# Two VectorE passes of a rational feed-forward stage joined over pairs of groups, with six buffers in place of four

## The chip, the cores and the metric

The kernel runs on one core of one Trainium2 chip. The metric is the time of one execution on the device, in microseconds (us). Of the core's engines TensorE (PE in the profile) multiplies matrices, VectorE (DVE) and ScalarE (ACT) work element by element, GpSimd (POOL) does so as well and also issues some of the DMAs, and SyncE (SP) issues the others.

## The reference, cut to what matters

The input has 4 x 3008 tokens of 256 values. A Fourier transform along the tokens, a complex 256x256 mix with a soft threshold, and the inverse transform come first. Each of the 12032 resulting tokens then goes through a feed-forward layer whose activation is a quotient of two polynomials:

```python
h = x @ w_in                       # 256 -> 2048
P = a[0] + a[1]*h + a[2]*h**2 + a[3]*h**3
Q = 1.0 + abs(b[0])*abs(h) + abs(b[1])*h**2
g = P / (Q + 1e-06)
out = g @ w_out                    # 2048 -> 256
```

## The kernel before

The feed-forward layer is cut into 26 tiles of 470 tokens (the last has 282). Each tile has eight groups, and a group is 256 of the 2048 hidden values, held as 128 partitions x 940 numbers. Groups are numbered through, 0 to 207. Every engine runs a loop over slots `q`; a slot handles one group at each step, and different steps of one slot belong to different groups. Each engine's order is written out by hand, and semaphores tie the engines together.

The steps of group r are these:

- PE, `group_f1` (L541): 12 matmuls at L552 make h in PSUM, in one of two buffers. It runs in PE's slot r-2 and waits for `n_n3` of group r-2, since VectorE must be done with that buffer.
- ACT, `group` (L770), in ACT's slot r-1: `den` = |h| scaled (L776), `sq` = h squared, scaled (L779), `num` (L782). The first waits until the remainder of group r-4 is done (`n_rest`), the second until `g_lo` of group r-4 is done (`n_g`), as the buffers come round after four groups.
- POOL, `tail` (L1135): a DMA adds `sq` to `den` (L1140). In ACT's slot r, L846 and L849 turn the sum into 1/Q, which goes into `sq`.
- DVE, in its slot r: L1087 and L1090 finish the numerator but for its constant. Both read h from PSUM. In slot r+1, `rounded` (L1056, its operation at L1062) makes `g_hi`, the quotient rounded to the format of the second matmul.
- DVE, in slot r+2: `multiplied` (L1065, at L1067) makes g_hi times the denominator, in `den`. `remainder` (L1071, at L1073) subtracts that from the numerator, in `num`. The order in a slot q is L1087 and L1090 for q, L1067 for q-2, L1062 for q-1, L1073 for q-2.
- POOL, in slot r+3: `g_lo` = num x sq (L1148), after the DMA of group r+3 in POOL's order and before that of group r+4.
- PE, in slot r+3: `group_f2_hi` (L567, L569) and `group_f2_lo` (L582) add g_hi and g_lo times w_out. `g_hi` has three buffers and `g_lo` two.

Up to about slot 141 the engines also carry the rest of the transform. PE has L469 to L493 for that. ACT has L722, L739 (`below`, which makes `neg`) and L750. DVE has `lower_x` (L945, L948), `soft` (L954, which reads `neg` and stands after L1073 in even slots), and twice a chain of small operations on the scales (slots 88 and 142). In the slots 1 and 3 of each tile PE does the last inverse step at L529. ACT reads it a slot later, at L762, or at L759 in the last tiles. `split_lo` (L1022) follows on DVE.

## Time and profile before

| | |
|---|---|
| median of 3 runs | 1445.55 us (1444.42 to 1447.71) |
| profiled execution | 1446.29 us, of which its span is 1444.1 us |
| busy share of the span | PE 96%, DVE 92%, ACT 87%, POOL 44% |
| mean granted TensorE clock | 0.991 |

The busy shares are over the whole span, and the stages have different limits. The prediction therefore reads two stretches by themselves. The first is DVE's slots 80 to 142, from 674.87 to 1081.37 us, in which the transform's work still runs. The second is slots 143 to 197, from 1081.37 to 1389.00 us, with the feed-forward layer and the inverse step alone. A slot starts where L1087 starts. In the timeline the columns are the start in us, the duration in us, the engine, line and operation, what it writes and reads with its size, and in brackets the idle time before it with what ended it. A waiting matmul or operation is shown from its start on, so a wait inside an operation makes it longer.

### The profile page before, as it was taken

How to read it: one execution, taken by the hardware profiler on the slowest of the kernel's cores; microseconds unless marked ns; L12 is line 12 of the kernel's file. 1: busy time of each engine (PE TensorE's matmuls, PEld its weight loads, DVE VectorE, ACT ScalarE, POOL GpSimd, SP SyncE). 2: the span in 40 equal slices, each digit the busy share in tenths (PEclk: the TensorE clock that was granted, in tenths of full speed). 3: DMA queues.
4: the chain of work that ended last, by engine and by line, in shares of the span. 5: the costliest groups of instructions: out<-in, count | busy, mean ns of one | idle time of the engine just before them, and what ended most of it. 6: DMA issues, size and time to landing. Idle time of an engine off the chain costs nothing.

```text
span 1444.1 us, 21576 instructions
## 1 busy us (share of the span) xinstructions
PE 1391.0 (96%) x7498; PEld 974.2 (67%) x7498; DVE 1333.8 (92%) x1650; ACT 1251.6 (87%) x1657; POOL 632.8 (44%) x417
## 2 busy tenths in 40 slices
PE   7998999999999999999999999999999999999987
PEld 2776667677666676776767776776766666666666
DVE  5576989989999999999999999999999999999998
ACT  3577989988989889888889989988989999999986
POOL 0000544444445444444445445545445555555554
PEclk8999999999999999999999999999999999999999
DMA  8885666666456656555555555555545555555443
GB/s 260 250 266 142 146 156 138 135 140 150 102 118 154 146 112 140 128 115 122 121 108 127 121 113 118 129 111 111 114 109 108 107 94 112 117 108 110 86 97 70
DMA packets 97913, 188.07 MB, mean 130 GB/s; under 512 B 11216, under 2 KB 57744, under 8 KB 97808
## 3 DMA queue, kind: packets, MB, share of 16 engines
q0 software_dynamic: 29952, 98.58, 36.8%
q1 hardware_dynamic: 67856, 88.12, 20.7%
q8 instruction: 62, 1.02, 0.3%
q14 instruction: 43, 0.35, 0.1%
HBM read 50.60 MB, written 37.49 MB: 61 GB/s over the span
## 4 chain that ended last, share of the span: by engine, by line
PE 53%; DVE 19%; ACT 16%; issue 8%; DMA 2%; POOL 1%; SPq 0%; ACTq 0%; DVEq 0%; POOLq 0%
PE h_ps L552 18%; PE o_ps L582 6%; PE o_ps L567 6%; PE o_ps L569 6%; DVE den L1067 4%; DVE num L1073 4%; DVE num L1087 4%; DVE g_hi L1062 4%; PE d L529 3%; ACT num L782 3%; ACT sq L779 3%; ACT den L776 3%; ACT sq L846 3%; PE d L493 2%; PE o_ps L463 2%
## 5 line engine op out<-in xcount | busy, mean ns | idle before, releaser
L1148 POOL TENSOR_TENSOR g_lo<-num,sq 128x940 fp32r<-128x940 f32 (+1 forms) x205 | 469.5, 2290 | 99.7 <-DVE num L1073 99.5
L1140 POOL DMA_DIRECT2D den<-sq x208 | 182.8, 879 | 698.9 <-ACT sq L779 369.0
L567 PE MATMUL o_ps<-g_hi,wout_hi 128*128 128x470 f32 (+1 forms) x832 | 342.1, 412 | 0.9 <-DVE g_hi L1062 0.9
L569 PE MATMUL o_ps<-g_hi,wout_lo 128*128 128x470 f32 (+1 forms) x832 | 310.5, 374 | 0.0
L552 PE MATMUL h_ps<-yt_hi,win_hi 128*128 128x470 f16 (+1 forms) x832 | 301.9, 363 | 5.3 <-DVE num L1090 5.3
L552 PE MATMUL h_ps<-yt_hi,win_lo 128*128 128x470 f16 (+1 forms) x832 | 300.1, 361 | 0.0
L552 PE MATMUL h_ps<-yt_lo,win_hi 128*128 128x470 f16 (+1 forms) x832 | 300.1, 361 | 0.0
L1087 DVE TENSOR_TENSOR num<-h_ps,num 128x940 f32<-128x940 f32 (+1 forms) x208 | 232.1, 1116 | 33.8 <-ACT num L782 33.0
L1090 DVE SCALAR_TENSOR_TENSOR num<-num,coef,h_ps 128x940 f32<-128x940 f32 (+1 forms) x208 | 245.2, 1179 | 7.4
L1067 DVE SCALAR_TENSOR_TENSOR den<-den,g_hi 128x940 f32<-128x940 f32 (+1 forms) x208 | 244.2, 1174 | 0.1
L1062 DVE SCALAR_TENSOR_TENSOR g_hi<-num,a_sb,sq 128x940 fp32r<-128x940 f32 (+1 forms) x208 | 244.3, 1174 | 0.0
L1073 DVE SCALAR_TENSOR_TENSOR num<-num,a_sb,den 128x940 f32<-128x940 f32 (+1 forms) x208 | 244.2, 1174 | 0.1
L779 ACT ACTIVATE sq<-h_ps,coef 128x940 f32<-128x940 f32 (+1 forms) x208 | 214.8, 1033 | 27.4 <-POOL g_lo L1148 26.2
L582 PE MATMUL o_ps<-g_lo,wout_hi 128*128 128x470 f32 (+1 forms) x832 | 213.8, 379 | 21.8 <-POOL g_lo L1148 21.0
L782 ACT ACTIVATE num<-h_ps,coef 128x940 f32<-128x940 f32 (+1 forms) x208 | 234.5, 1127 | 0.0
L846 ACT ACTIVATE sq<-den,qone 128x940 f32<-128x940 f32 (+1 forms) x208 | 223.8, 1076 | 3.9 <-DMA den<-sq 3.8
L776 ACT ACTIVATE den<-h_ps,coef 128x940 f32<-128x940 f32 (+1 forms) x208 | 213.2, 1025 | 5.8 <-DVE num L1073 4.2
L849 ACT ACTIVATE sq<-sq 128x940 f32<-128x940 f32 (+1 forms) x208 | 203.2, 977 | 6.6
L582 PEld LDWEIGHTS o_ps<-g_lo,wout_hi 128*128 128x128 f32 x832 | 152.2, 189 | 56.5 <-POOL g_lo L1148 37.6
L567 PEld LDWEIGHTS o_ps<-g_hi,wout_hi 128*128 128x128 f32 x832 | 157.9, 190 | 30.9 <-issue 8.3
L569 PEld LDWEIGHTS o_ps<-g_hi,wout_lo 128*128 128x128 f32 x832 | 158.0, 190 | 23.5 <-issue 7.5
L552 PEld LDWEIGHTS h_ps<-yt_hi,win_hi 128*128 128x128 f16 x832 | 81.2, 98 | 115.4 <-issue 47.9
(161 smaller groups left out, 1581.1 us busy)
## 6 DMA issues: line engine op xcount, KB each, us to landing
den<-sq POOLq DMA_DIRECT2D x200, 470.0 KB, 4.4
spec<-s1w SPq DMA_DIRECT2D x64, 192.0 KB, 2.8
z_in<-spec SPq DMA_DIRECT2D x96, 128.0 KB, 2.6
spec<-s_out SPq DMA_DIRECT2D x96, 128.0 KB, 1.9
xw<-in_x SPq DMA_DIRECT2D x31, 384.0 KB, 4.8
out_t<-o_sb SPq DMA_DIRECT2D x25, 470.0 KB, 4.2
zp_in<-spec SPq DMA_DIRECT2D x22, 480.0 KB, 5.4
inv_in<-in_inv SPq DMA_DIRECT2D x96, 64.0 KB, 2.3
```

The lines of the kernel that those rows point to most:

```text
L552: mm = pe.matmul(h_ps[q % 2][:, j, 0:cols(q)], w[:, h, f * P:(f + 1) * P], y[t % 2][:, h, 0:cols(q)], start=i == 0, stop=i == len(terms) - 1)
L567: pe.matmul(o_ps[:, h, 0:w], wout_hi[:, f, h * P:(h + 1) * P], g_hi[q % 3][:, j, 0:w], start=f == 0, stop=False)
L569: mm = pe.matmul(o_ps[:, h, 0:w], wout_lo[:, f, h * P:(h + 1) * P], g_hi[q % 3][:, j, 0:w], start=False, stop=False)
L582: mm = pe.matmul(o_ps[:, h, 0:w], wout_hi[:, f, h * P:(h + 1) * P], g_lo[q % 2][:, j, 0:w], start=False, stop=f == FB - 1)
L779: act.activation(ring(sq, q), h, ACT.Square, scale=scales(q // SLOTS, 3)).then_inc(n_sq, 1)
L782: act.activation(ring(num, q), h, ACT.Identity, bias=scales(q // SLOTS, 4), scale=scales(q // SLOTS, 5)).then_inc(n_num, 1)
L846: act.activation(ring(sq, q), ring(den, q), ACT.Abs_reciprocal_sqrt, bias=qone[:, 0:1]).then_inc(n_rs, 1)
L1062: dve.scalar_tensor_tensor(out=g_hi[r % 3][:, :, 0:w], in0=ring(num, r), scalar=a_sb[:, 0:1], in1=ring(sq, r), op0=ALU.add, op1=ALU.mult). ...
L1067: dve.scalar_tensor_tensor(out=ring(den, r), in0=ring(den, r), scalar=1.0 + 1e-6, in1=g_hi[r % 3][:, :, 0:cols(r)].bitcast(F32), op0=ALU.a ...
L1073: dve.scalar_tensor_tensor(out=ring(num, r), in0=ring(num, r), scalar=a_sb[:, 0:1], in1=ring(den, r), op0=ALU.add, op1=ALU.subtract).then_ ...
L1087: dve.tensor_tensor(top, h, top, ALU.mult).then_inc(n_n2, 1)
L1148: pool.tensor_tensor(g_lo[r % 2][:, :, 0:cols(r)], ring(num, r), ring(sq, r), ALU.mult).then_inc(n_g, 1)
```

## The change

For the groups 80 to 197 (`PAIRED`), L1067 and L1073 become one operation each for two groups, an even one and the next odd one, with 1880 numbers in each partition. The product of the pair r, r+1 stands at the end of DVE's slot r+2, behind `rounded(r+1)`, whose result it reads, and behind `split_lo` and `soft`. The remainder of the pair stands in slot r+3, after L1090 and `lower_x` and before `rounded(r+2)`. The second matmul and `g_lo` of a paired group come one slot later, in slot r+4. `num`, `den` and `sq` have six buffers from group 80 on. Two of each lie in the space of the inputs `x` and of the first transform's output, which are no longer used by then; two waits check this. `g_hi` has four buffers in place of three for all groups. A small start-up buffer is shared with `neg`, and `pick` becomes bf16.

```diff
+PAIRED = range(80, 198)
 def f2_slot(r):
+    if r in PAIRED:
+        return r + 4
     return r + 3 if late(r) else r + 2
+def place(q):
+    return q % 4 if q < PAIRED[0] else (q - PAIRED[0] + 4) % 6
...
-                done = [r for r in (q - 3, q - 2) if 0 <= r < NS and f2_slot(r) == q]
+                done = [r for r in (q - 4, q - 3, q - 2) if 0 <= r < NS and f2_slot(r) == q]
...
-                if q >= 4:
-                    act.wait_ge(n_rest, q - 3)
+                before = user_before(q)
...
+                if before is not None:
+                    act.wait_ge(n_rest, back_steps(before))
...
-                if r >= 3:
-                    dve.wait_ge(f2h, r - 2)
+                if r >= 4:
+                    dve.wait_ge(f2h, r - 3)
...
+            def multiplied_pair(r):
+                dve.wait_ge(n_hi, r + 2)
+                dve.scalar_tensor_tensor(out=both(den_pairs, r), in0=both(den_pairs, r), scalar=1.0 + 1e-6,
+                                         in1=g_hi_pairs[r // 2 % 2][:, :, :].bitcast(F32),
+                                         op0=ALU.add, op1=ALU.mult).then_inc(n_back, 1)
+            def remainder_pair(r):
+                dve.wait_ge(n_back, back_steps(r))
+                dve.scalar_tensor_tensor(out=both(num_pairs, r), in0=both(num_pairs, r), scalar=a_sb[:, 0:1],
+                                         in1=both(den_pairs, r), op0=ALU.add, op1=ALU.subtract).then_inc(n_rest, 1)
...
-                if 0 <= q - 2 < NS and late(q - 2):
+                if 0 <= q - 2 < NS and late(q - 2) and q - 2 not in PAIRED:
                     multiplied(q - 2)
...
+                if q - 3 in PAIRED and q % 2 == 1:
+                    remainder_pair(q - 3)
                 if 0 <= q - 1 < NS:
                     rounded(q - 1)
...
+                if q - 2 in PAIRED and q % 2 == 0:
+                    multiplied_pair(q - 2)
...
-                for r in [r for r in (q - 3, q - 2) if 0 <= r < NS and f2_slot(r) == q and not on_vector(r)]:
-                    pool.wait_ge(n_rest, r + 1)
+                for r in [r for r in (q - 4, q - 3, q - 2) if 0 <= r < NS and f2_slot(r) == q and not on_vector(r)]:
+                    pool.wait_ge(n_rest, back_steps(r))
```

## Rows read from the trace of the kernel before

**Rows 1.** Busy time by stretch; columns: stretch, length, engines' busy time, clock, DMA share, GB/s.
```profile
674.87:1081.37 406.50, 399.84 (x2215) 287.03 (x2213) 392.73 (x481) 360.92 (x452) 194.53 (x126) 1.00 0.54 117
1081.37:1389.00 307.63, 297.39 (x1457) 197.04 (x1458) 305.03 (x277) 287.86 (x310) 170.24 (x110) 0.99 0.53 105
```

**Rows 2.** Chain that ended last, shares by line, 674.87 to 1081.37 us.
```profile
by line: PE h_ps L552 24.2%; PE o_ps L582 8.7%; PE o_ps L567 8.5%; PE o_ps L569 8.4%; issue 5.9%; PE d L529 4.8%; ACT num L782 4.0%; ACT den L776 3.9%; ACT sq L779 3.7%; ACT sq L846 3.4%; PE d L469 2.0%; PE d L493 1.9%; DVE num L1073 1.7%; 
```

**Rows 3.** The same, 1081.37 to 1389.00 us.
```profile
by line: issue 15.9%; DVE den L1067 13.4%; DVE num L1073 13.0%; DVE g_hi L1062 12.6%; DVE num L1087 12.2%; PE h_ps L552 6.8%; POOL g_lo L1148 4.3%; ACT num L782 4.0%; ACT sq L779 3.8%; ACT den L776 2.8%; PE o_ps L582 2.7%; PE d L529 2.1%; A
```

**Rows 4.** Timeline of DVE, slot 168 and the start of 169.
```profile
1221.39 1.13 DVE L1087 TENSOR_TENSOR num<-h_ps,num 128x940 f32<-128x940 f32 x1
1222.55 1.19 DVE L1090 SCALAR_TENSOR_TENSOR num<-num,coef,h_ps 128x940 f32<-128x940 f32 x1
1223.66 1.13 DVE L1067 SCALAR_TENSOR_TENSOR den<-den,g_hi 128x940 f32<-128x940 f32 x1
1224.71 1.19 DVE L1062 SCALAR_TENSOR_TENSOR g_hi<-num,a_sb,sq 128x940 fp32r<-128x940 f32 x1
1225.82 1.19 DVE L1073 SCALAR_TENSOR_TENSOR num<-num,a_sb,den 128x940 f32<-128x940 f32 x1
1226.92 1.13 DVE L1087 TENSOR_TENSOR num<-h_ps,num 128x940 f32<-128x940 f32 x1
```

**Rows 5.** Groups of DVE by shape, from 1081.37 us; last column: busy us, mean ns.
```profile
L1073 DVE SCALAR_TENSOR_TENSOR num<-num,a_sb,den 128x940 f32<-128x940 f32 x60 | 71.4, 1190 | 0.0
L1073 DVE SCALAR_TENSOR_TENSOR num<-num,a_sb,den 128x564 f32<-128x564 f32 x8 | 6.4, 797 | 0.1
```

**Rows 6.** Timeline of POOL in slot 168.
```profile
1221.56 2.22 POOL L1148 TENSOR_TENSOR g_lo<-num,sq 128x940 fp32r<-128x940 f32 x1 [0.82 <-DVE num L1073]
1225.41 0.88 POOL L1140 DMA_DIRECT2D den<-sq  x1 [1.63 <-PE o_ps L582]
```

**Rows 7.** Timeline of PE in slot 168: L582, first and last matmul of L552.
```profile
1223.83 1.12 PE L582 MATMUL o_ps<-g_lo,wout_hi 128*128 128x470 f32 x4 [0.30 <-POOL g_lo L1148]
1224.79 0.37 PE L552 MATMUL h_ps<-yt_hi,win_hi 128*128 128x470 f16 x1
...
1226.98 0.36 PE L552 MATMUL h_ps<-yt_hi,win_lo 128*128 128x470 f16 x1
```

**Rows 8.** Timeline of ACT in slot 168.
```profile
1222.24 1.03 ACT L776 ACTIVATE den<-h_ps,coef 128x940 f32<-128x940 f32 x1
1223.81 1.05 ACT L779 ACTIVATE sq<-h_ps,coef 128x940 f32<-128x940 f32 x1 [0.54 <-POOL g_lo L1148]
```

**Rows 9.** Timeline of POOL near 538 us.
```profile
537.92 0.90 POOL L1140 DMA_DIRECT2D den<-sq  x1 [5.25 <-issue]
538.53 2.51 POOL L1148 TENSOR_TENSOR g_lo<-num,sq 128x940 fp32r<-128x940 f32 x1
```

**Rows 10.** Timeline of DVE near 540 us.
```profile
540.00 2.05 DVE L1067 SCALAR_TENSOR_TENSOR den<-den,g_hi 128x940 f32<-128x940 f32 x1
```

**Rows 11.** Timeline of DVE at a tile's slot 4, in the second stretch.
```profile
1201.31 1.33 DVE L1067 SCALAR_TENSOR_TENSOR den<-den,g_hi 128x940 f32<-128x940 f32 x1
```

**Rows 12.** Timeline of ACT at a tile's slot 4, in the first stretch.
```profile
861.00 0.48 ACT L739 ACTIVATE neg<-d,x_lam 128x256 f32<-128x256 f32 x1
```

**Rows 13.** Timeline of DVE in the same slot, 108, and the next.
```profile
861.60 0.42 DVE L954 SCALAR_TENSOR_TENSOR ythr<-d,neg 128x256 f32<-128x256 f32 x1 [0.35 <-ACT neg L739]
...
862.63 1.14 DVE L1087 TENSOR_TENSOR num<-h_ps,num 128x940 f32<-128x940 f32 x1 [0.59 <-ACT num L782]
```

**Rows 14.** Timeline of PE: the first L552 of slot 109.
```profile
866.42 0.37 PE L552 MATMUL h_ps<-yt_hi,win_hi 128*128 128x470 f16 x1
```

**Rows 15.** Waits in the first stretch; columns: us in total, times, longest.
```profile
PEld d L529 <- ACT s_out L750: 6.3, 8, 2.0
```

**Rows 16.** Timeline of PE in slot 83: the first L567 and the first L552.
```profile
694.68 0.46 PE L567 MATMUL o_ps<-g_hi,wout_hi 128*128 128x470 f32 x1
...
697.33 0.37 PE L552 MATMUL h_ps<-yt_hi,win_hi 128*128 128x470 f16 x1
```

More of the change, by code:

```diff
@@ L158, in on_vector, with back_steps, user_before @@
     return r >= NS - 3
+PAIRED = range(80, 198)
 def f2_slot(r):
+    if r in PAIRED:
+        return r + 4
     return r + 3 if late(r) else r + 2
+def back_steps(r):
+    pairs = sum(1 for s in PAIRED if s % 2 == 1 and s < r)
+    return r + 1 - pairs - (r in PAIRED and r % 2 == 1)
+def place(q):
+    return q % 4 if q < PAIRED[0] else (q - PAIRED[0] + 4) % 6
+def user_before(q):
+    if q < PAIRED[0]:
+        return q - 4 if q >= 4 else None
+    return q - 6 if q >= PAIRED[0] + 2 else None
 LATE_TILES = range(ENTRY[-1], NT)
@@ L237, in spectral_ffn @@
         neg = sb("neg", P, D)
+        bias_rest = neg
         ythr, s4_out = several("ythr", 2, P, D), several("s4_out", 2, P, D)
@@ L240, in spectral_ffn @@
         yt_hi, yt_lo = several("yt_hi", 2, P, KH, 480, dt=F16), several("yt_lo", 2, P, KH, 480, dt=F16)
-        num, sq, den = (several(n, 4, P, GB * BANK) for n in ("num", "sq", "den"))
-        g_hi, g_lo = several("g_hi", 3, P, GB, TOK, dt=F32R), several("g_lo", 2, P, GB, TOK, dt=F32R)
+        num_pairs, den_pairs = [several(n, 2, P, 2, GB * BANK) for n in ("num", "den")]
+        num_pairs.append(xw[:, 0:2, :, :].rearrange("p i a d -> p i (a d)"))
+        den_pairs.append(xw[:, 2:4, :, :].rearrange("p i a d -> p i (a d)"))
+        num, den = ([pair[:, i, :] for pair in pairs for i in range(2)] for pairs in (num_pairs, den_pairs))
+        sq = [t[:, :] for t in several("sq", 4, P, GB * BANK)]
+        sq += [s1w[:, 2 * i:2 * i + 2, :].rearrange("p i d -> p (i d)") for i in range(2)]
+        g_hi_pairs, g_lo = several("g_hi", 2, P, 2, GB * TOK, dt=F32R), several("g_lo", 2, P, GB, TOK, dt=F32R)
+        g_hi = [pair[:, i, :].rearrange("p (j n) -> p j n", j=GB) for pair in g_hi_pairs for i in range(2)]
         o_sb = several("o_sb", 2, P, KH, TOK)
@@ L301, in ring, with both @@
         def ring(tiles, q):
-            return tiles[q % 4][:, 0:GB * cols(q)].rearrange("p (j n) -> p j n", j=GB)
+            return tiles[place(q)][:, 0:GB * cols(q)].rearrange("p (j n) -> p j n", j=GB)
+        def both(pairs, q):
+            return pairs[place(q) // 2][:, :, 0:GB * cols(q)]
         zp_count = []
@@ L566, in group_f2_hi @@
                     for h in range(KH):
-                        pe.matmul(o_ps[:, h, 0:w], wout_hi[:, f, h * P:(h + 1) * P], g_hi[q % 3][:, j, 0:w],
+                        pe.matmul(o_ps[:, h, 0:w], wout_hi[:, f, h * P:(h + 1) * P], g_hi[q % 4][:, j, 0:w],
                                   start=f == 0, stop=False)
-                        mm = pe.matmul(o_ps[:, h, 0:w], wout_lo[:, f, h * P:(h + 1) * P], g_hi[q % 3][:, j, 0:w],
+                        mm = pe.matmul(o_ps[:, h, 0:w], wout_lo[:, f, h * P:(h + 1) * P], g_hi[q % 4][:, j, 0:w],
                                        start=False, stop=False)
@@ L773, in group @@
                 act.wait_ge(f1, q + 1)
-                if q >= 4:
-                    act.wait_ge(n_rest, q - 3)
+                before = user_before(q)
+                if q in PAIRED and before is None:
+                    act.wait_ge(p1, B * S1N)
+                    act.wait_ge(x_act, B * S1N - FRONT_S1)
+                    for i in range(4):
+                        act.wait_ge(s_st1[i], B * S1N // 4 * 16)
+                if before is not None:
+                    act.wait_ge(n_rest, back_steps(before))
                 act.activation(ring(den, q), h, ACT.Abs, scale=scales(q // SLOTS, 2)).then_inc(n_den, 1)
-                if q >= 4:
-                    act.wait_ge(n_g, q - 3)
+                if before is not None:
+                    act.wait_ge(n_g, before + 1)
                 act.activation(ring(sq, q), h, ACT.Square, scale=scales(q // SLOTS, 3)).then_inc(n_sq, 1)
@@ L1059, in rounded @@
                 dve.wait_ge(n_n3, r + 1)
-                if r >= 3:
-                    dve.wait_ge(f2h, r - 2)
-                dve.scalar_tensor_tensor(out=g_hi[r % 3][:, :, 0:w], in0=ring(num, r), scalar=a_sb[:, 0:1], in1=ring(sq, r),
+                if r >= 4:
+                    dve.wait_ge(f2h, r - 3)
+                dve.scalar_tensor_tensor(out=g_hi[r % 4][:, :, 0:w], in0=ring(num, r), scalar=a_sb[:, 0:1], in1=ring(sq, r),
                                          op0=ALU.add, op1=ALU.mult).then_inc(n_hi, 1)
@@ L1113, in _ @@
                     split_lo(S5_AT[q - 1], d0[:, :])
-                if 0 <= q - 2 < NS and late(q - 2):
+                if 0 <= q - 2 < NS and late(q - 2) and q - 2 not in PAIRED:
                     remainder(q - 2)
@@ L1139, in tail @@
                 pool.wait_ge(n_sq, q + 1)
[L1140 removed]
+                pool.dma_start(den[place(q)][:, 0:w], sq[place(q)][:, 0:w], accum_op=ALU.add).then_inc(s_q[q % 4], 16)
             tail(0)
             for q in range(NS + 2):
[L1144 to L1145 removed]
+                for r in [r for r in (q - 4, q - 3, q - 2) if 0 <= r < NS and f2_slot(r) == q and not on_vector(r)]:
+                    pool.wait_ge(n_rest, back_steps(r))
                     if r >= 2:
```

13 lines of the change are left out of this document (6 added, 7 removed).

## The prediction

> **What bounds the kernel now.** I read the busy time by stretch first, then the chain of waits of each stretch, then the timelines of single slots. From slot 80 to 142, PE is busy for 399.84 of 406.50 us and DVE for 392.73 [rows 1], and the chain runs over PE's matmuls [rows 2]. PE bounds this stretch, with DVE close behind. From slot 143 to 197, DVE is busy for 305.03 of 307.63 us, PE for 297.39 and ACT for 287.86 [rows 1]. The chain runs over DVE's five operations in turn [rows 3]. In slot 168 they follow each other without a gap, and the slot takes 1226.92 - 1221.39 = 5.53 us [rows 4]. So one microsecond of DVE is worth one microsecond in the second stretch and little in the first.
>
> **What a pair saves on DVE.** An operation of L1073's kind takes 1190 ns for 940 numbers and 797 ns for 564 [rows 5], which is 393/376 = 1.045 ns a number. The 940 numbers that are added then cost 0.98 us. From start to start, L1067 takes 1224.71 - 1223.66 = 1.05 us and L1073 1226.92 - 1225.82 = 1.10 us [rows 4]. What is paid for each operation and not for its numbers is thus 0.07 us at L1067 and 0.12 us at L1073. A pair saves 0.19 us.
>
> The product of the pair now stands directly behind the operation whose result it reads. L1090 stands so behind L1087: from start to start that takes 1222.55 - 1221.39 = 1.16 us, where L1067, as long as L1087, takes 1.05 [rows 4]. Such a neighbour costs 0.11 us, once a pair. Net 0.08 us for two slots. The bounds of this term are 0.19 us (if the wait costs nothing) and 0 (if a long operation pays more). I take 0.08, since L1087 and L1090 are the same case.
>
> The second stretch and the paired slots behind it hold 28 pairs, so 28 x 0.08 = 2.2 us, between 0 and 5.3.
>
> **What deeper buffers save.** 55 slots of 5.53 us make 304.2 us, and the stretch takes 307.6 [rows 1]. 3.4 us lie in waits at the tiles' starts, where ACT has extra work and runs late. One of them is a product stretched from 1.13 to 1.33 us [rows 4, 11]. With six buffers ACT no longer waits for `g_lo` (0.54 us in slot 168 [rows 8]) and comes into these slots with a lead, but POOL's work at these places can still be late. Between 0 and 3.4 us; I take the middle, 1.7.
>
> **The first stretch.** PE idles 406.50 - 399.84 = 6.7 us in 63 slots [rows 1], of which up to 6.3 us are waits of L529 for ACT's L750 [rows 15]. The change takes no work from ACT, and L750 stands at the end of ACT's slot, so I expect nothing of this. The bounds are 0 and 6.7 us.
>
> Against it stands the place of `soft`. It comes before the product of the pair now, and it waits for ACT. In slot 108, `neg` is done at 861.00 + 0.48 = 861.48, `soft` starts at 861.60 and the next slot at 862.63 [rows 12, 13]. With the pair behind `soft`, DVE needs 0.34 us for it (0.42 less the 0.08 of overlap that [rows 4] show) and 1.05 + 0.98 = 2.03 us for the pair. Slot 109 then starts at 861.60 + 0.34 + 2.03 = 863.97, 1.34 us later. L1090 of slot 109 ends 2.35 us on, at 866.32. PE's L552 waits for that and started at 866.42 [rows 14]. The 1.34 us just fit. I count 0.1 us for each of seven tiles, 0.7 us in all; the bounds are 0 and the rival below.
>
> **What is moved.** The second matmul comes a slot later. In slot 83 PE therefore has none, and its 2.65 us before L552 (694.68 to 697.33 [rows 16]) fall away there and come back in slot 201, where two groups end together. In slot 201 PE waits for `g_lo` of group 198 in both kernels, so the added matmuls of group 197 can lie in that wait. I count -0.5 us at slot 83 and nothing at the end, with up to 2.65 us either way. POOL keeps its count of operations and DMAs. The waits on the old users of the borrowed space cost nothing: the last of these works in slot 70. SP's order does not change but for the outputs, a slot later, with a buffer to spare.
>
> **The sum.** -2.2 - 1.7 + 0.7 - 0.5 = -3.7 us. 1446.29 us, the profiled execution (span 1444.1), becomes 1442.6. It stood 0.74 us above the median, so the median becomes 1441.8 us.
>
> **The rival that decides: POOL and DVE.** Before the change, `g_lo` starts 0.17 us into the slot, when the remainder is done, and ends at 2.39 [rows 4, 6]. That is beside L1087 and L1090, which take one input from PSUM. L1067 takes both from SBUF, and where `g_lo` is late L1067 stands still. Near 540 us `g_lo` ends at 541.04 and L1067 at 542.05, after 2.05 us in place of 1.13 [rows 9, 10]. So L1067 does nearly all its work only when `g_lo` is done. All three of L1067, L1062 and L1073 take both inputs from SBUF.
>
> Two `g_lo` fall to each pair, and their remainder is one operation. For the even group, `g_lo` becomes free inside the odd slot while `rounded` runs. It should go behind it, into the even slot's first 2.3 us, where it costs nothing. For the odd group nothing of DVE holds `g_lo` back any more. It starts when POOL has issued the next DMA, which depends on ACT's L779. That can be in the even slot between `rounded` and the product of the pair, at the point where DVE waits for its own result.
>
> The times in an even slot, counted from its start, are these. `rounded` starts at 2.27 (where L1067 stood [rows 4]) and lasts 1.19, to 3.46. The pair's product starts at 2.27 + 1.11 + 0.11 = 3.49. PE's L582 waits for `g_lo` as now, so L552 starts 3.40 us into the slot before and ends at 1227.34 - 1221.39 = 5.95 [rows 7], which is 0.48 into this slot. L776 and L779 need 1.03 + 1.05 less 0.1 of overlap [rows 8], to 2.46. The DMA starts 1225.41 - 1224.86 = 0.55 us behind that [rows 6, 8], at 3.01, and `g_lo` 0.61 us behind the DMA [rows 9], at 3.62. The product is first, by 0.13 us. If it is, `g_lo` waits for it and goes into the next odd slot, beside L1087 and L1090, and nothing is lost. If it is not, `g_lo` runs from 3.46 to 5.67, the product ends 1.01 + 0.98 later, at 7.66, and the next slot starts at 7.58 in place of 5.52. That is 2.06 us a pair.
>
> Each case keeps itself up. With an early `g_lo`, PE's L582 and L552 and with them ACT and the DMA are a microsecond earlier two slots on. At slots 2 and 4 of each tile, ACT's extra read delays L779, and there the product is first. So about two pairs of the four of each tile can collide: 14 x 2.06 = 29 us less the 3.7 won, 1471 us. All 28 would be 58 us, and about 1500. No row shows POOL waiting for DVE; that is the open point.
>
> The Trainium skill (SBUF — State Buffer, Who interferes with whom) says that a VectorE operation with two SBUF inputs and a GpSimd operation that reads SBUF shut each other out for a whole instruction, and that the order of issue decides. By that rule the waits of [rows 10] are as they should be, and the rival costs what I gave; it also says that DVE can hold POOL off, which no row here shows.
>
> **The other rivals.** DVE's lag in the first stretch may not fit. The slots 2 and 4 of each tile have `soft` late. The price of each is 1.3 us of DVE, and it decides from the point at which L1090 ends after PE's 866.42. Both in full for seven tiles make 18 us, and 1460; half of it 1451. The opposite is that ACT's lead takes PE's waits away, 6.7 us of them, for 1435. Or the two small gains are given back at the tiles' starts: 1444 to 1447.
>
> **How the numbers follow.** Forecast, 1441.8 us (1437 to 1445): 40 in 100, of which 33 are faster by over 0.2%. PE's waits go too, 1435: 10. Gains given back: 10. DVE's lag bounds the first stretch, 1451: 12, of which 2 stay within 0.2%. POOL collides with the product, 1471 and up: 28. Faster by over 0.2% (2.9 us, about what the measurement can tell) is 33 + 10 = 43; the same 7 + 10 + 2 = 19; slower 10 + 28 = 38. The range takes in the forecast and most of the middle of the collision case, from 1435 to 1478; the cases that are left out are all pairs colliding and a gain above 10 us.
>
> **What would show it.** The pair's product should take 2.1 us and the remainder 2.17. If the product shows more than 3 us and `g_lo` starts inside even slots after 3.4 us, the rival holds. In the second stretch the sum of an even and an odd slot should be 11.0 us in place of 11.07. ACT's waits for `g_lo` should be gone. In slot 108, slot 109 should start about 9.0 us after it. The prediction is wrong if POOL does not wait for DVE, if a long operation costs more than its numbers, or if PE's L552 waits for L1090 in the first stretch for more than 0.2 us a tile.

## The result and the profile after

| | before | after |
|---|---|---|
| median | 1446.63 us (1444.42 to 1449.45, 4 runs) | 1542.34 us (1527.81 to 1548.22, 4 runs) |
| ratio to before | | 1.0646 [1.0564, 1.0727] |
| profiled execution | 1446.29 us (span 1444.1) | 1548.22 us (span 1546.4) |
| mean granted TensorE clock | 0.991 | 0.975 |

The change makes the kernel 6.5% slower. The forecast of 1441.8 us was wrong and the range of 1435 to 1478 us doesn't hold the time. The case that came is the one that the prediction called the deciding rival, POOL against VectorE, but larger than it was worked out, and for the most part in a stretch for which it wasn't worked out at all.

The lines of the kernel have moved. L1138 and L1141 are what L1087 and L1090 were, L586 and L616 of PE what L552 and L582 were, L1102 is `rounded` (L1062), L1113 the product of a pair, L1119 the remainder of a pair, L1203 is `g_lo` (L1148) and L1195 the DMA ahead of it (L1140). L994 is `soft` (L954), L773 makes `neg` (L739), L819 is the second of ACT's three reads of h (L779). The buffers four and five of `num` and `den` appear as `xw` and those of `sq` as `s1w`. The page of the kernel after, busy time and chain of its whole span:

```profile
PE 1419.1 (92%) x7498; PEld 981.1 (63%) x7498; DVE 1418.9 (92%) x1532; ACT 1249.1 (81%) x1657; POOL 687.8 (44%) x417
...
PE 42%; DVE 35%; ACT 13%; issue 7%; DMA 2%; POOL 1%; ACTq 0%; SPq 0%; DVEq 0%; POOLq 0%
```

VectorE has fewer operations than before and is busy longer. The page alone doesn't say where. I cut each profiled execution at the starts of VectorE's slots 80, 143 and 199, so that the stretches hold the same groups in every kernel (us):

| profiled execution of | to slot 80 | slots 80 to 142 | 143 to 198 | 199 to the end | all |
|---|---|---|---|---|---|
| before | 674.9 | 406.5 | 313.1 | 49.6 | 1444.1 |
| after | 672.9 | 489.7 | 332.4 | 51.4 | 1546.4 |

83.2 us are lost in the first stretch, 19.3 in the second, 1.8 at the end. Busy time of each engine in the two stretches of the kernel after, with columns as in [rows 1] (the view is cut 0.33 us behind the starts of the slots, at the same lengths):

```profile
673.26:1162.97 489.71, 422.29 (x2205) 291.11 (x2202) 458.84 (x419) 365.05 (x456) 223.00 (x127) 0.95 0.45 97
1162.97:1495.34 332.37, 308.57 (x1490) 203.75 (x1490) 328.35 (x225) 291.00 (x315) 199.13 (x112) 0.98 0.50 100
```

In the first stretch VectorE has 419 operations in place of 481 and is busy for 458.84 us in place of 392.73 [rows 1]. PE, which bounded this stretch, now idles for 489.71 - 422.29 = 67.4 us, where it had 6.7. Its granted clock fell from 1.00 to 0.95. The table has PE's busy time 22 us up for practically the same matmuls, so part of the loss of clock stretches PE's work, but PE no longer sets the end there. The groups of VectorE by shape, over the whole span of the kernel after (last columns: busy us, mean ns, idle before):

```profile
L1113 DVE SCALAR_TENSOR_TENSOR den<-den,g_hi 128x1880 f32<-128x1880 f32 x39 | 123.2, 3158 | 0.7
L1113 DVE SCALAR_TENSOR_TENSOR xw<-xw,g_hi 128x1880 f32<-128x1880 f32 x20 | 65.1, 3254 | 0.3
...
L1102 DVE SCALAR_TENSOR_TENSOR g_hi<-num,a_sb,sq 128x940 fp32r<-128x940 f32 x160 | 212.1, 1326 | 0.5 <-ACT sq L889 0.5
L1119 DVE SCALAR_TENSOR_TENSOR num<-num,a_sb,den 128x1880 f32<-128x1880 f32 x39 | 85.4, 2189 | 0.0
```

The pair's product takes 3.16 and 3.25 us on average, where 2.1 was expected, and the roundings take 1.33 in place of 1.19. The pair's remainder takes its 2.19. A mean hides two kinds. Single products take either 2.11 or 4.3 to 4.9 us, and nothing between. Slot 108 shows one of the second kind. First VectorE, then POOL, then ACT, in the timeline of the kernel after:

```profile
893.95 1.19 DVE L1102 SCALAR_TENSOR_TENSOR g_hi<-num,a_sb,sq 128x940 fp32r<-128x940 f32 x1
...
898.15 0.42 DVE L994 SCALAR_TENSOR_TENSOR ythr<-d,neg 128x256 f32<-128x256 f32 x1 [1.62 <-ACT neg L773]
...
898.50 4.81 DVE L1113 SCALAR_TENSOR_TENSOR den<-den,g_hi 128x1880 f32<-128x1880 f32 x1
903.23 1.12 DVE L1138 TENSOR_TENSOR num<-h_ps,num 128x940 f32<-128x940 f32 x1
```

```profile
898.21 0.88 POOL L1195 DMA_DIRECT2D den<-sq  x1 [4.35 <-PE o_ps L616]
898.82 2.50 POOL L1203 TENSOR_TENSOR g_lo<-xw,s1w 128x940 fp32r<-128x940 f32 x1
...
911.55 0.88 POOL L1195 DMA_DIRECT2D xw<-s1w  x1
912.16 2.48 POOL L1203 TENSOR_TENSOR g_lo<-num,sq 128x940 fp32r<-128x940 f32 x1
```

```profile
896.62 1.04 ACT L819 ACTIVATE sq<-h_ps,coef 128x940 f32<-128x940 f32 x1
897.55 0.48 ACT L773 ACTIVATE neg<-d,x_lam 128x256 f32<-128x256 f32 x1
```

VectorE waits 1.62 us for `neg`, starts the product at 898.50 and ends it at 903.31, 1.99 us after `g_lo` ends at 901.32. That is [rows 9, 10] again on a long operation: the product does its work only when `g_lo` is done. The slot starts at 891.68 and the next at 903.23, so it lasts 11.55 us. POOL's last two lines belong to slot 110. There `g_lo` of the even group ran from 908.42 on, and the next DMA and the next `g_lo` stood right behind it. The rounding beside them was the one held:

```profile
911.63 4.01 DVE L1102 SCALAR_TENSOR_TENSOR g_hi<-num,a_sb,sq 128x940 fp32r<-128x940 f32 x1
```

Counted over single operations of the profiled execution after, in us beyond an undisturbed product (2.11) or rounding (1.19):

| | pairs | products held | roundings held |
|---|---|---|---|
| slots 80 to 142 | 31 | 17, +45.0 | 8, +22.7 |
| slots 143 to 198 | 28 | 8, +18.7 | 1, +2.7 |

In the first stretch this makes 67.7 us, and two small operations on the scales (slots 88 and 142) were held by 2.7 and 2.5 us. That is 72.9 us. VectorE's busy time went up by 458.84 - 392.73 = 66.1 us. The 6.8 between them are about what the pairs save in busy time (e11 below, in which no product is held, has 392.73 - 387.94 = 4.8 us less than before), and 2 us are left over. The rest of the 83.2 us is VectorE's idle time, 30.9 us in place of 13.8. Its largest part is a wait that came with the change, in the view of waits of the first stretch (in total, times, longest), with PE's waits for VectorE above it:

```profile
PEld h_ps L586 <- DVE num L1141: 48.6, 18, 3.8
...
DVE ythr L994 <- ACT neg L773: 19.1, 14, 1.6
```

In the second stretch VectorE is busy for 328.35 us where the kernel before had 310.46 in the same slots. These 17.9 us are the 21.4 us of the table less 3.5 for the pairs (e11 below, with no product and one rounding held, the rounding by 0.6 us, is busy for 306.16 us, 4.3 less than before). The 1.8 us at the end are one rounding more, in slot 200 (VectorE, then POOL):

```profile
1503.56 3.11 DVE L1102 SCALAR_TENSOR_TENSOR g_hi<-num,a_sb,sq 128x940 fp32r<-128x940 f32 x1
```

```profile
1503.20 2.47 POOL L1203 TENSOR_TENSOR g_lo<-num,sq 128x940 fp32r<-128x940 f32 x1
```

So the time after is accounted for to within 2 us. What decides who is held, and what opened the first stretch to it, was for the experiments.

### The profile page after: what moved, and what is told of

Read it like the earlier page. It is cut to its first block, busy times and chain, and to the rows that moved or that the text cites. A ratio compares the mean times of both kernels' runs of the same rounds, so it can differ in the third digit from the quotient of the medians.

```text
span 1546.4 us, 21462 instructions
## 1 busy us (share of the span) xinstructions
PE 1419.1 (92%) x7498; PEld 981.1 (63%) x7498; DVE 1418.9 (92%) x1532; ACT 1249.1 (81%) x1657; POOL 687.8 (44%) x417
## 3 DMA queue, kind: packets, MB, share of 16 engines
q1 hardware_dynamic: 67856, 88.12, 19.3%
## 4 chain that ended last, share of the span: by engine, by line
PE 42%; DVE 35%; ACT 13%; issue 7%; DMA 2%; POOL 1%; ACTq 0%; SPq 0%; DVEq 0%; POOLq 0%
PE h_ps L586 16%; DVE g_hi L1102 7%; DVE den L1113 7%; PE o_ps L616 4%; DVE num L1138 4%; PE o_ps L601 4%; PE o_ps L603 4%; DVE xw L1113 4%; PE d L563 3%; DVE num L1119 3%; ACT den L816 3%; ACT sq L819 2%; DVE xw L1138 2%; DVE num L1141 2%; PE d L527 2%
## 5 line engine op out<-in xcount | busy, mean ns | idle before, releaser
L1203 POOL TENSOR_TENSOR g_lo<-num,sq 128x940 fp32r<-128x940 f32 (+1 forms) x163 | 420.7, 2581 | 116.2 <-DVE num L1119 83.6
L1195 POOL DMA_DIRECT2D den<-sq x164 | 143.7, 876 | 593.8 <-ACT sq L819 316.1
L586 PE MATMUL h_ps<-yt_hi,win_hi 128*128 128x470 f16 (+1 forms) x832 | 312.5, 376 | 90.8 <-DVE num L1141 64.7
L586 PE MATMUL h_ps<-yt_lo,win_hi 128*128 128x470 f16 (+1 forms) x832 | 310.9, 374 | 0.0
L586 PE MATMUL h_ps<-yt_hi,win_lo 128*128 128x470 f16 (+1 forms) x832 | 310.2, 373 | 0.0
L616 PE MATMUL o_ps<-g_lo,wout_hi 128*128 128x470 f32 (+1 forms) x832 | 214.1, 380 | 12.8 <-POOL g_lo L1203 12.1
L586 PEld LDWEIGHTS h_ps<-yt_hi,win_hi 128*128 128x128 f16 x832 | 83.2, 100 | 211.9 <-DVE num L1141 75.8
L1102 DVE SCALAR_TENSOR_TENSOR g_hi<-num,a_sb,sq 128x940 fp32r<-128x940 f32 (+1 forms) x164 | 215.3, 1313 | 0.5 <-ACT sq L889 0.5
L1138 DVE TENSOR_TENSOR num<-h_ps,num 128x940 f32<-128x940 f32 (+1 forms) x164 | 183.9, 1121 | 26.4 <-ACT num L822 26.1
L1141 DVE SCALAR_TENSOR_TENSOR num<-num,coef,h_ps 128x940 f32<-128x940 f32 (+1 forms) x164 | 194.2, 1184 | 5.9
L822 ACT ACTIVATE num<-h_ps,coef 128x940 f32<-128x940 f32 (+1 forms) x164 | 186.0, 1134 | 0.0
L816 ACT ACTIVATE den<-h_ps,coef 128x940 f32<-128x940 f32 (+1 forms) x164 | 168.8, 1029 | 19.1 <-PE h_ps L586 18.7
L616 PEld LDWEIGHTS o_ps<-g_lo,wout_hi 128*128 128x128 f32 x832 | 152.6, 190 | 47.2 <-POOL g_lo L1203 28.7
L886 ACT ACTIVATE sq<-den,qone 128x940 f32<-128x940 f32 (+1 forms) x164 | 177.5, 1082 | 1.8 <-DMA den<-sq 1.8
L819 ACT ACTIVATE sq<-h_ps,coef 128x940 f32<-128x940 f32 (+1 forms) x164 | 169.6, 1034 | 2.5 <-POOL g_lo L1203 2.5
L889 ACT ACTIVATE sq<-sq 128x940 f32<-128x940 f32 (+1 forms) x164 | 160.8, 980 | 5.2
L586 PEld LDWEIGHTS h_ps<-yt_hi,win_lo 128*128 128x128 f16 x832 | 84.0, 101 | 88.1 <-issue 12.2
L1203 POOL TENSOR_TENSOR g_lo<-xw,s1w 128x940 fp32r<-128x940 f32 (+1 forms) x42 | 116.8, 2780 | 50.3 <-DVE xw L1119 48.8
```

Source lines behind the costliest of these rows:

```text
L586: mm = pe.matmul(h_ps[q % 2][:, j, 0:cols(q)], w[:, h, f * P:(f + 1) * P], y[t % 2][:, h, 0:cols(q)], start=i == 0, stop=i == len(terms) - 1)
L616: mm = pe.matmul(o_ps[:, h, 0:w], wout_hi[:, f, h * P:(h + 1) * P], g_lo[q % 2][:, j, 0:w], start=False, stop=f == FB - 1)
L816: act.activation(ring(den, q), h, ACT.Abs, scale=scales(q // SLOTS, 2)).then_inc(n_den, 1)
L819: act.activation(ring(sq, q), h, ACT.Square, scale=scales(q // SLOTS, 3)).then_inc(n_sq, 1)
L822: act.activation(ring(num, q), h, ACT.Identity, bias=scales(q // SLOTS, 4), scale=scales(q // SLOTS, 5)).then_inc(n_num, 1)
L886: act.activation(ring(sq, q), ring(den, q), ACT.Abs_reciprocal_sqrt, bias=qone[:, 0:1]).then_inc(n_rs, 1)
```

## The experiments

The stretches of every kernel, cut as above (us, from the profiled executions):

| | to slot 80 | 80 to 142 | 143 to 198 | 199 to the end | all |
|---|---|---|---|---|---|
| before | 674.9 | 406.5 | 313.1 | 49.6 | 1444.1 |
| after | 672.9 | 489.7 | 332.4 | 51.4 | 1546.4 |
| e1_reads_nothing | 670.7 | 412.5 | 308.2 | 46.6 | 1438.1 |
| e2_before_reads_nothing | 670.1 | 406.9 | 310.2 | 46.5 | 1433.8 |
| e3_hold | 673.1 | 419.6 | 311.0 | 51.4 | 1455.1 |
| e4_soft_behind | 673.6 | 416.6 | 325.9 | 50.9 | 1467.0 |
| e5_hold_soft_behind | 671.7 | 407.6 | 311.0 | 50.9 | 1441.2 |
| e6_from_144 | 674.5 | 406.5 | 333.0 | 51.0 | 1465.0 |
| e7_two_ops | 674.7 | 496.8 | 375.0 | 51.7 | 1598.2 |
| e8_hold_from_144 | 676.4 | 408.2 | 311.1 | 50.9 | 1446.6 |
| e9_buffers_only | 675.9 | 406.6 | 313.7 | 49.3 | 1445.5 |
| e10_hold_rounded | 673.0 | 407.1 | 308.8 | 50.8 | 1439.6 |
| e11_hold_rounded_again | 672.7 | 407.2 | 309.3 | 51.1 | 1440.3 |
| e12_pairs_to_189 | 675.1 | 407.2 | 311.6 | 49.6 | 1443.4 |

### Is it POOL's reads?

In both kernels the product `g_lo` is replaced by an operation that only writes. e1 is the kernel after, e2 the kernel before with the same edit.

```
-  pool.tensor_tensor(g_lo[r % 2][:, :, 0:cols(r)], ring(num, r), ring(sq, r), ALU.mult).then_inc(n_g, 1)
+  pool.memset(g_lo[r % 2][:, :, 0:cols(r)].bitcast(F32), 0.0).then_inc(n_g, 1)
```

> The changed kernel, in which GpSimd fills g_lo with zeros and reads nothing (the multiplication num x sq is left out). Theory of the lock: VectorE's operations with two SBUF inputs are held only by a GpSimd operation that reads SBUF, so no product of a pair takes more than 2.2 us and no rounding more than 1.3 us, and the time falls from 1548 to between 1425 and 1450 us. Rival, the new order itself (the product behind soft, the second matmul a slot later): the 4.8 us products stay or become idle time of the same length, and the time stays above 1500 us.

> The kernel before with the same edit (GpSimd fills g_lo with zeros), as the control for e1_reads_nothing. Theory of the lock: before the change GpSimd hardly stood in VectorE's way, so at most 10 us are gained: 1435 to 1446 us. Rival, that taking out GpSimd's work is worth as much anywhere: over 30 us are gained here too.

Measured: e1 1440.13 us and e2 1436.19 (one run each). Nothing is held in e1. The product has the mean of an undisturbed one in every pair, and so has the rounding (groups of e1 by shape):

```profile
L1113 DVE SCALAR_TENSOR_TENSOR den<-den,g_hi 128x1880 f32<-128x1880 f32 x39 | 82.4, 2114 | 0.7
...
L1102 DVE SCALAR_TENSOR_TENSOR g_hi<-num,a_sb,sq 128x940 fp32r<-128x940 f32 x160 | 190.6, 1191 | 0.0
```

Where POOL reads nothing, the change costs 4 us, and not 96. The order of work, the deeper buffers and the long operations are the same in e1 as after, so the reads of `g_lo` beside VectorE are what costs. The operation that only writes is also shorter, 1.21 us in place of 2.2, in e1 and e2 alike; that a shorter POOL is not what helps is shown by e3 and e10 below, in which all of `g_lo`'s work is done. e2 shows what e1 shows of the rest. In the first stretch the change costs 412.5 - 406.9 = 5.6 us without any operation held. In the second it gains 2.0. The 5.6 us show as waits of PE for VectorE in the first stretch, 6.0 us in all (0.6 in e2), of which this line of e1's view of waits has 5.7. That is the lag that `soft` brings, with what the passage to pairs costs in slots 82 to 85:

```profile
PE h_ps L586 <- DVE num L1141: 5.7, 3, 3.0
```

### Taking `g_lo` out of the way by an order

e3 lets POOL's `g_lo` of the odd group wait until the next pair's product is done. e4 leaves that out and moves the pair's product ahead of `soft`. e5 is both.

```
 e3, in POOL's loop, ahead of g_lo
+  if r in PAIRED and r % 2 == 1 and r + 1 in PAIRED:
+      pool.wait_ge(n_back, back_steps(r + 1))
 e4, in VectorE's loop
+  if q - 2 in PAIRED and q % 2 == 0:
+      multiplied_pair(q - 2)
   if q - 2 in S2_AT:
...
-  if q - 2 in PAIRED and q % 2 == 0:
-      multiplied_pair(q - 2)
```

> The changed kernel and one more wait: GpSimd issues g_lo of an odd group only when the product of the pair behind it is done (n_back). All work is there. Theory of the lock: g_lo of the odd groups then runs beside L1138 and L1141, nothing is stretched, and the time is 1438 to 1455 us, the forecast of the prediction for the case without collisions plus the lag of the first stretch. Rival, the new order or the long operations cost the time: one more wait can only add, and the time stays at 1530 us or more.

> The changed kernel with soft behind the product of the pair in even slots, and no added wait. Theory of the lock, with GpSimd's DMA as the point that decides: in the slots 2 and 4 of each tile of the first stretch the product starts 2 to 3 us earlier and is ahead of the DMA, so the products of 4.8 us vanish there; the other even slots keep a rounding or a product held for 2 to 2.8 us. Slots 80 to 142 take 430 to 465 us in place of 490, the whole 1490 to 1525 us. Rival, that the place of soft alone is to blame: the time is that of e5_hold_soft_behind, 1445 us.

> As e3_hold, with soft behind the product of the pair in even slots in place of ahead of it. If the place of soft costs VectorE its 1.3 us in the slots 2 and 4 of the first stretch and they reach PE, this is 3 to 18 us faster than e3_hold; if the lag fits beside PE's work, as the prediction had it, the two are within 3 us.

Measured: e3 1455.96 us, ratio 1.0059 [1.0042, 1.0076]. e4 1469.82, ratio 1.0166 [1.0148, 1.0184]. e5 1445.31, ratio 0.9993 [0.9983, 1.0003].

e3 holds no product. This group of e3 answers to the 3158 ns of the kernel after:

```profile
L1113 DVE SCALAR_TENSOR_TENSOR den<-den,g_hi 128x1880 f32<-128x1880 f32 x39 | 82.5, 2115 | 0.7
```

Its first stretch is still 13 us longer than before. Moving `soft` behind the product brings 419.6 to 407.6 us, so the place of `soft` costs 12 us in e3. VectorE's wait for `neg` is in the view of waits of e3's first stretch, with the largest wait of PE below it; the same view of e5 has no line for `neg`:

```profile
DVE ythr L994 <- ACT neg L773: 22.6, 15, 1.6
PE o_ps L616 <- POOL g_lo L1205: 12.8, 14, 1.9
```

The 12 us are not the lag by itself. In e1 VectorE waits for `neg` for 19.2 us, nearly as long, and the stretch is only 5.6 us longer than that of e2. What e3 has on top is its own wait: `g_lo` is kept back until the late product is done, and PE waits for `g_lo`.

e4 missed its expectation by far, to the good. I had given most of the loss to POOL's order of work, which e4 doesn't touch. Yet the first stretch fell from 489.7 to 416.6 us, with no product and no rounding held in it. The slot that took 11.55 us shows why (slot 108 of e4, VectorE, then POOL):

```profile
864.65 2.11 DVE L1113 SCALAR_TENSOR_TENSOR den<-den,g_hi 128x1880 f32<-128x1880 f32 x1
866.68 0.42 DVE L994 SCALAR_TENSOR_TENSOR ythr<-d,neg 128x256 f32<-128x256 f32 x1
```

```profile
866.41 0.88 POOL L1195 DMA_DIRECT2D den<-sq  x1 [4.52 <-PE o_ps L616]
```

The product is nearly over when the DMA starts. In the kernel after, `soft` waits for `neg`, and `neg` follows L819 directly on ACT. L819 also releases POOL's DMA. Both engines thus set off from the same event: the DMA starts 898.21 - 897.66 = 0.55 us behind L819's end, the product 0.84 us behind it. POOL is ahead by 0.29 us each time. Without `soft` in front, VectorE is ahead by 1.76 us. What remains in e4's first stretch against e5 is 9.0 us. Two small operations on the scales are held by 2.7 and 2.8 us (L1041 in slot 88 takes 2.90 in place of 0.22 us, L1151 in slot 142 3.04 in place of 0.27), and slots 90 and 132 to 133 are 2.3 and 1.6 us longer. The second stretch keeps 7 products held, +16.2 us.

### Is the first stretch needed for the second?

e6 pairs only from group 144 on, e8 is e6 with the wait of e3.

```
-PAIRED = range(80, 198)
+PAIRED = range(144, 198)
```

> The changed kernel with the pairs and the six buffers from group 144 on in place of 80. If four fifths of the loss come from the first stretch, as the trace says (83 of 102 us), this takes 1450 to 1470 us. If a loss of the same size per pair arises wherever pairs are, it takes 1490 us or more.

> Pairs and six buffers from group 144 on, with the wait of e3_hold. The first stretch is that of the kernel before (406 us), the second that of e3_hold (311 us in place of 313). Theory of the lock and the sum of 0.08 us a pair: 1 to 3 us faster than the kernel before, 1443 to 1445 us.

Measured: e6 1466.94 us, ratio 1.0141 [1.0126, 1.0156], as expected. Its first stretch is that of before, and its second has 8 products held, +18.7 us, the same number as after. So the collisions of the second stretch don't come from a state carried over from the first. e8 1446.49, ratio 1.0003 [0.9994, 1.0012]: the wait takes the 20 us away, but the gain of some 2 us that was expected isn't there. The second stretch is 2.0 us shorter (311.1), and the first is 1.7 and the end 1.3 longer. The first has the same work as in e6, where it took 406.5, so that part is within the spread of executions; at the end a rounding is held by 1.9 us, as in the kernel after.

### Is a long operation at fault?

e7 makes two operations of 940 numbers out of each long one, in the place of the long one.

```
-  dve.scalar_tensor_tensor(out=both(den_pairs, r), in0=both(den_pairs, r), scalar=1.0 + 1e-6,
...
+  for s in (r, r + 1):
+      op = dve.scalar_tensor_tensor(out=ring(den, s), in0=ring(den, s), scalar=1.0 + 1e-6,
...
```

> The changed kernel with two operations of 940 numbers in the place of each long one, in the same order and with the same buffers. Theory of the lock: the loss is in the order and not in the length; the first of the two products is held as the long one was, and 59 x 0.19 us come on top: 1530 to 1575 us. Rival, that an operation of 1880 numbers is what goes wrong: under 1480 us.

Measured: 1600.35 us (one run), worse than expected and worse than the change. In slot 162 of e7 the first product and the DMA start together, 0.03 us apart (VectorE, then POOL):

```profile
1298.79 4.18 DVE L1114 SCALAR_TENSOR_TENSOR den<-den,g_hi 128x940 f32<-128x940 f32 x2
```

```profile
1298.76 0.88 POOL L1199 DMA_DIRECT2D den<-sq  x1 [1.26 <-PE o_ps L616]
1299.36 2.62 POOL L1207 TENSOR_TENSOR g_lo<-xw,s1w 128x940 fp32r<-128x940 f32 x1
```

The two products take 4.18 us together. Each begins anew, and `g_lo` goes between them. A long operation that is first keeps POOL out for all its length; two short ones don't. So the length isn't at fault. It halves the number of places at which VectorE can lose: 36 of e7's 118 short products are held, where 25 of 59 long ones were.

### What decides who is first

The prediction measured by the start of `g_lo` in the records. Slot 144 and slot 168 of the kernel after show that this is the wrong mark. The product and POOL's lines of slot 144, then of slot 168:

```profile
1171.60 2.12 DVE L1113 SCALAR_TENSOR_TENSOR den<-den,g_hi 128x1880 f32<-128x1880 f32 x1
...
1310.06 4.41 DVE L1113 SCALAR_TENSOR_TENSOR den<-den,g_hi 128x1880 f32<-128x1880 f32 x1
```

```profile
1171.51 0.88 POOL L1195 DMA_DIRECT2D den<-sq  x1 [1.22 <-PE o_ps L616]
1172.12 3.68 POOL L1203 TENSOR_TENSOR g_lo<-xw,s1w 128x940 fp32r<-128x940 f32 x1
...
1309.39 0.88 POOL L1195 DMA_DIRECT2D den<-sq  x1 [0.64 <-ACT sq L819]
1309.99 2.49 POOL L1203 TENSOR_TENSOR g_lo<-xw,s1w 128x940 fp32r<-128x940 f32 x1
```

In slot 144 the DMA is 0.09 us ahead of the product, the product takes its 2.12 us, and `g_lo` takes 3.68 and ends 2.08 us after it. This time POOL waited for VectorE. In slot 168 the DMA is 0.67 us ahead and the product waits. Slot 108 lies between: the product starts 0.32 us before the record of `g_lo`, and still waits, since the DMA was 0.29 us ahead. Over all 59 pairs of both stretches the rule is this. Where `g_lo` stands directly behind the DMA (47 pairs), the product is held in all 25 in which the DMA starts 0.19 us or more before it, and in none of the 22 in which it starts 0.09 us before it (slot 144) or later. Where `g_lo` isn't queued behind the DMA (12 pairs), no product is held, even with the DMA 0.29 us ahead. The prediction's margin of 0.13 us from the record of `g_lo` is thus a lead of the DMA by 0.61 - 0.13 = 0.48 us, well beyond those 0.19.

Counted from the product's start, the mark doesn't fit the roundings. The eight that are held in the first stretch have the DMA only 0.07 to 0.08 us ahead of them (slot 110 above: 911.55 and 911.63), less than the 0.09 of slot 144. Their records start 0.08 us before the end of L1141's, while a product's starts 0.03 us after the end of the rounding's. Counted from the end of the operation ahead on VectorE, both fit. In the traces of the kernel after, e4, e6 and e7, slots 81 to 198, I took every product and rounding whose record overlaps by over 0.15 us with that of a `g_lo` queued directly behind its DMA. All 111 are held (take longer than alone) in which the DMA starts 0.08 us or more before that end, and none of the 68 in which it starts 0.06 us before it or later. Roundings directly behind a remainder aren't counted, since the remainder is what releases the `g_lo` beside them. The nearest on either side are slot 134 of e4 and slot 176 of e7, each as the rounding, the product behind it (in e7 both products in one line), and POOL's DMA:

```profile
1029.70 1.19 DVE L1102 SCALAR_TENSOR_TENSOR g_hi<-num,a_sb,sq 128x940 fp32r<-128x940 f32 x1
1030.92 2.12 DVE L1113 SCALAR_TENSOR_TENSOR den<-den,g_hi 128x1880 f32<-128x1880 f32 x1
1030.83 0.88 POOL L1195 DMA_DIRECT2D xw<-s1w  x1 [1.22 <-ACT s1w L819]
...
1392.16 1.19 DVE L1102 SCALAR_TENSOR_TENSOR g_hi<-num,a_sb,sq 128x940 fp32r<-128x940 f32 x1
1393.39 5.04 DVE L1114 SCALAR_TENSOR_TENSOR den<-den,g_hi 128x940 f32<-128x940 f32 x2
1393.27 0.88 POOL L1199 DMA_DIRECT2D xw<-s1w  x1 [1.19 <-ACT s1w L819]
```

e10 is a direct trial of "who is first". It has the order of e4, and the wait on POOL is for the rounding that also releases the product, and not for the product. Both engines are then let go by the same event, and nothing makes `g_lo` wait but VectorE's own start.

```
+  if r in PAIRED and r % 2 == 1:
+      pool.wait_ge(n_hi, r + 3)
```

> As e5_hold_soft_behind, but GpSimd is released by the end of the rounding (n_hi), the event that releases VectorE's product of the pair too. It asks who takes the port when both are let go at once. In the changed kernel's trace the product went first where GpSimd's DMA started up to 0.09 us ahead of it, so VectorE should win here and the time be 1440 to 1450 us; if GpSimd wins, 2.1 us a pair come on top, and it is 1550 us or more.

Measured: 1441.45 us (one run), as expected. Slot 152 of e10 (VectorE, then POOL):

```profile
1133.06 2.12 DVE L1113 SCALAR_TENSOR_TENSOR den<-den,g_hi 128x1880 f32<-128x1880 f32 x1
1135.09 1.13 DVE L1138 TENSOR_TENSOR xw<-h_ps,xw 128x940 f32<-128x940 f32 x1
```

```profile
1132.37 0.88 POOL L1195 DMA_DIRECT2D xw<-s1w  x1 [0.61 <-ACT s1w L819]
1133.17 4.09 POOL L1205 TENSOR_TENSOR g_lo<-num,sq 128x940 fp32r<-128x940 f32 x1
```

The product starts 0.11 us before `g_lo` and is not held; `g_lo` shows 4.09 us, of which it waits the first 2. The DMA's 0.69 us of lead does nothing here, since the wait stands between it and `g_lo`. No product is held in e10. In nine of its 59 pairs the two engines are let go together like this (slots 88, 142, 144 and every eighth from 152 to 192); in the others `g_lo` comes later by itself.

The Trainium skill (SBUF — State Buffer, Who interferes with whom) says that the two engines shut each other out for a whole instruction and that the order of issue decides. By that rule POOL can be held off too; the prediction had no row for that, and now there are the 3.68 us of slot 144 and the 4.09 us of e10. These runs agree with the rule, and they say which event of a queued POOL operation counts.

### What the deeper buffers bring, and the best version

e9 keeps the six buffers and the later places of the new waits but has the single operations in the old order. e11 is e10 again, timed. e12 is e10 with pairs to group 189.

```
-PAIRED = range(80, 198)
+PAIRED = range(80, 190)
```

> Six buffers and four of g_hi as in the changed kernel, but the operations of the kernel before, one group each, in their old order, and the second matmul in slot r+3. The prediction gave deeper buffers 0 to 3.4 us in the second stretch, 1.7 as the middle: 1441 to 1446 us. Rival, that the added buffers or their places do harm: over 1449 us.

> e10_hold_rounded once more, timed over five rounds, for it is the version that the experiments point to. By its trace the second stretch took 308.8 us in place of 313.1, the first 407.1 in place of 406.5 and the end 1.3 us more: 1441 to 1445 us, 0.1 to 0.4% faster than the kernel before. If the single run was chance, the ratio is 1 within 0.1%.

> As e11, but the last pair is 188 and 189 in place of 196 and 197, so that the slot in which two groups come to the second matmul lies among full slots where TensorE has room. If the 1.3 us more behind slot 199 come from that slot, they go, less 4 pairs x 0.08 us: about 1 us faster than e11. If not, it is 0 to 0.5 us slower.

Measured: e9 1446.53 us, ratio 1.0006 [0.9997, 1.0015]; e11 1442.2, ratio 0.9976 [0.9966, 0.9986]; e12 1443.35, ratio 0.9983 [0.9973, 0.9992].

e9 gains nothing, and its second stretch is as long as that of before (313.7 against 313.1 us). The waits at the tiles' starts, which I had meant the buffers to remove, are still there. A group of e9 by shape, from 1100 to 1350 us, shows what they are:

```profile
L1104 DVE SCALAR_TENSOR_TENSOR den<-den,g_hi 128x940 f32<-128x940 f32 x30 | 35.6, 1185 | 0.0
```

An undisturbed product takes 1.13 us, and these take 1.185 on average: they stand behind a `g_lo` that is late. The row of 1.33 us [rows 11], which I read as ACT running late, was a small case of the same lock. In e10 these slots last as long as all others but for slot 174, in which a rounding is held by 0.6 us; e11 keeps that one and 0.5 us in slots 148 and 149. The product has moved away from `g_lo`. ACT's waits for `g_lo`, 17.7 us over both stretches before, are gone in e9 as in the kernel after, and e9 shows that this brings nothing.

e11 is the best version of all, 0.24% faster than before and 6.5% than the change. Its second stretch is 3.8 us shorter than before (e10: 4.3), its first 0.7 longer and its end 1.5 longer. The end is a held operation too. Behind the last pair, `g_lo` meets a rounding of 564 numbers, which takes 0.79 us alone (timeline of e11 in slot 201, VectorE, then POOL):

```profile
1403.09 2.75 DVE L1102 SCALAR_TENSOR_TENSOR g_hi<-xw,a_sb,s1w 128x564 fp32r<-128x564 f32 x1
```

```profile
1399.12 6.12 POOL L1205 TENSOR_TENSOR g_lo<-num,sq 128x940 fp32r<-128x940 f32 x2 [1.47 <-issue]
```

In e12, where the pairs end earlier, the last stretch is 49.6 us again, as in before. But its second stretch is 2.3 us longer than e11's, more than the 1.5 that are won. Four pairs less account for 4 x 0.07 = 0.3 us, and the other 2.0 are one more held operation, at the passage from pairs to single ones. There two `g_lo` stand in a row on POOL, and the single product of slot 193, of 940 numbers, starts 0.14 us behind the second:

```profile
1360.83 3.11 DVE L1107 SCALAR_TENSOR_TENSOR den<-den,g_hi 128x940 f32<-128x940 f32 x1
```

```profile
1360.69 2.26 POOL L1205 TENSOR_TENSOR g_lo<-num,sq 128x940 fp32r<-128x940 f32 x1
```

## Why the prediction was wrong

**What bounds the kernel** was right as far as it went. PE's 6.7 us of idle time in the first stretch are no cover, though. VectorE idled there for 13.8 us only, and 83 us of held operations, waits and aftermath can't hide in that. The prediction took it that one microsecond of VectorE is worth "little in the first", as if that held for any amount.

**What a pair saves** was right. In e10 an odd slot takes 5.47 us and an even one 5.54, 11.01 a pair for the 11.0 of the prediction. The product takes 2.11 and the remainder 2.17. The second stretch of e10, where no product is held, is 4.3 us shorter, for 2.2 + 1.7 = 3.9 predicted.

**What deeper buffers save** was wrong in its reason, though the sum came out. e9 shows them to bring nothing. The waits went because the product no longer lies beside a late `g_lo`. In e3, e5 and e8, where `g_lo` is held until the product's end and then starts 0.23 us into a slot, part of them is still there and the stretch is 311.0 us.

**The first stretch** fails at its second step, the place of `soft`. The lag was put at 1.34 us in slot 108. In e3, with no product held, slot 108 lasts 8.25 us against 7.69 before, and slot 106 lasts 8.78 against 7.45. It was said to fit beside PE, for 0.7 us in all. It costs up to 5.6 us by e1 against e2, where PE waits for L1141 for 6.0 us in place of 0.6, a third of the rival's 18 us; with the held-back `g_lo` of e3 on top it is 12 us. The larger part is what the step didn't ask. By waiting for `neg`, the product was tied to the same event on ACT that releases POOL's DMA, 0.29 us behind it. The prediction had every number for this. With [rows 12, 13], the product would start 0.48 + 0.12 + 0.34 = 0.94 us after `neg` starts. `neg` starts 0.1 us before the end of L779 (the overlap that the prediction took for ACT's records), and with [rows 6, 8] the DMA starts 0.55 behind that end, 0.65 us after `neg` starts. The DMA is ahead by 0.29 us, as measured. I worked the race out for the second stretch only. Taking `soft` away from in front of the product (e4) brings the whole from 1542 to 1470 us.

**What is moved** was put at -0.5 us at slot 83 and nothing at the end. The gain at slot 83 isn't there: slots 82 to 85 take 27.81 us in e10, 1.13 more than before, and VectorE waits for ACT's L756 for 1.9 us in them. The end is 1.2 to 1.8 us longer in the versions with pairs to group 197 (2.1 in e7), within the bound of 2.65. It is one rounding held by 1.9 or 2.0 us (slot 200 or 201). In e1, where nothing is held, the end is as long as in e2 (46.6 and 46.5 us), so the moved matmuls themselves cost nothing, as predicted.

**The rival** had the right mechanism and the right places in the second stretch, and about half the frequency: 8 of 28 pairs are held, where it gave 14 if it came. Its open point, whether POOL waits for VectorE, came out as it had assumed: the even group's `g_lo`, let go while the rounding runs, takes 3.1 us in place of 2.2 (3.14 in slot 109, from 908.42) and goes behind it. Its price was too low: 2.3 us in slot 168 (4.41 - 2.12) to 2.7 in slot 108 in place of 2.06, since VectorE also waits for the rest of the DMA. The step that failed is the one that set the chance, "`g_lo` 0.61 us behind the DMA [rows 9], at 3.62. The product is first, by 0.13 us". It took the record's start of `g_lo` for the moment at which POOL takes the memory. When `g_lo` is queued behind the DMA, the race is over by then: POOL wins from a start of the DMA 0.08 us before the end of VectorE's last operation. By that mark the prediction's own numbers, 3.01 for the DMA against 3.46 for the rounding's end, say that the product is held. With the right mark the forecast would have been the rival.

**That a case keeps itself up** held in the first stretch. VectorE, slowed, bounds it, so ACT and POOL are early, POOL's next DMA stands ready when the even group's `g_lo` ends, and the next `g_lo` goes ahead of a rounding (slot 110). Eight roundings were lost like that; none is held in e4's first stretch.

What stays open: why the mark lies where it does, between 0.06 and 0.08 us ahead of the end of VectorE's operation; why the kernel after varies by 20 us from run to run where before varies by 5 (races decided by tenths of a microsecond would do that, but this isn't shown); and what makes VectorE wait longer for ACT in slots 82 to 85. How much of PE's lower clock in the first stretch added to the time wasn't tried by itself.
